# A gated linear attention and two dense layers: attention outputs from block two on in 64x64 array tiles, packed into x by DMAs, and low parts of weight pieces moved to VectorE

## What is computed

```python
for t in range(S):
    state = alpha[:, :, t, :, None] * state + einsum('bhd,bhe->bhde', k[:, :, t], v[:, :, t])
    y[:, :, t] = einsum('bhd,bhde->bhe', q[:, :, t], state)
x = y.transpose(0, 2, 1, 3).reshape(B * S, H * D)
x = mish-like gate of (x @ w_in), times w_out      # h * tanh(softplus(h))
x = (x @ w_in2) * cos(x @ w_in2), times w_out2
```

## Time and profile before

| | |
|---|---|
| median of 3 runs | 884.51 us |
| profiled execution | 883.49 us, span 881.8 us |
| PE busy | 869.1 us, 99% of the span |
| DVE, ACT, POOL busy | 437.2, 405.6, 367.9 us |
| mean granted TensorE clock | 0.998 |
| HBM traffic | 64 GB/s over the span |

### The profile page before, as it was taken

The page is one execution under the profiler, slowest core; times in us unless marked ns, Lnnn a source line. Parts: engine busy times, 40 slices in busy tenths (PEclk is TensorE's granted clock), DMA queues, the critical chain, the costliest instruction groups (busy, mean ns, idle before and its releaser), DMA issues.

```text
span 881.8 us, 16421 instructions
## 1 busy us (share of the span) xinstructions
PE 869.1 (99%) x6614; PEld 719.2 (82%) x6614; DVE 437.2 (50%) x674; ACT 405.6 (46%) x697; POOL 367.9 (42%) x283
## 2 busy tenths in 40 slices
PE   8989999999999999999999999999999999999998
PEld 7768888888888888888888788888888888888886
DVE  8895533333433333320022766665666666666564
ACT  3634333232223223223454765655656556565554
POOL 3786654444455444342455333332333323233232
PEclk9999999999999999999999999999999999999999
DMA  9646543334334333510233200200200200200000
GB/s 222 197 111 161 137 103 72 83 67 110 83 63 108 72 80 66 122 33 1 69 129 90 72 1 1 72 0 1 72 1 1 72 1 1 72 1 1 36 1 36
DMA packets 65611, 57.79 MB, mean 66 GB/s; under 512 B 41952, under 2 KB 51168, under 8 KB 65536
## 3 DMA queue, kind: packets, MB, share of 16 engines
q1 hardware_dynamic: 65536, 56.75, 24.7%
HBM read 42.57 MB, written 14.16 MB: 64 GB/s over the span
## 4 chain that ended last, share of the span: by engine, by line
PE 93%; DVE 4%; issue 1%; ACT 1%; DMA 0%; POOL 0%; ACTq 0%; DVEq 0%; POOLq 0%
PE low L569 43%; PE low L546 33%; PE pair L546 11%; PE top L506 1%; DVE suffix L772 1%; PE top L487 1%; PE pair L439 1%; PE top L492 1%; PE low L466 1%; DVE w_lo L861 1%; DVE growth L783 1%; DMA shared<-aqk_in 0%; DVE probs L816 0%; ACT w_hi L621 0%; PE pair L466 0%
## 5 line engine op out<-in xcount | busy, mean ns | idle before, releaser
L981 POOL TENSOR_TENSOR g_lo<-g,g_hi 128x512 fp32r<-128x512 f32 x192 | 260.4, 1357 | 465.0 <-ACT g_hi L671 465.0
L569 PE MATMUL low<-g_hi,w_hi 128*128 128x512 f32 x576 | 224.6, 390 | 0.3 <-DVE x_out L877 0.3
L569 PE MATMUL low<-g_hi,w_lo 128*128 128x512 f32 x576 | 224.1, 389 | 0.0
L671 ACT ACTIVATE g_hi<-g 128x512 fp32r<-128x512 f32 x192 | 120.7, 628 | 117.6 <-PE low L569 116.8
L569 PE MATMUL low<-g_lo,w_hi 128*128 128x512 f32 x576 | 165.7, 389 | 0.0
L569 PEld LDWEIGHTS low<-g_hi,w_hi 128*128 128x128 f32 x576 | 108.1, 188 | 23.7 <-DVE x_out L877 0.7
L569 PEld LDWEIGHTS low<-g_lo,w_hi 128*128 128x128 f32 x576 | 108.1, 188 | 22.6
L569 PEld LDWEIGHTS low<-g_hi,w_lo 128*128 128x128 f32 x576 | 108.1, 188 | 22.3
L546 PE MATMUL low<-x_hi,w_hi 128*128 128x512 f32 x432 | 124.7, 397 | 0.4 <-ACT x_hi L635 0.3
L546 PE MATMUL low<-x_hi,w_lo 128*128 128x512 f32 x432 | 122.0, 391 | 0.0
L546 PE MATMUL low<-x_lo,w_hi 128*128 128x512 f32 x432 | 121.4, 389 | 0.0
(11 more groups left out here) (108 smaller groups left out, 912.3 us busy)
## 6 DMA issues: line engine op xcount, KB each, us to landing
w_raw<-w_in SPq DMA_DIRECT2D x32, 384.0 KB, 3.3
shared<-aqk_in SPq DMA_DIRECT2D x44, 192.0 KB, 3.8
v_sb<-v_in SPq DMA_DIRECT2D x24, 256.0 KB, 4.3
shared<-aqk_in SPq DMA_DIRECT2D x48, 96.8 KB, 2.7
turned<-x_out SPq DMA_DIRECT2D x72, 64.0 KB, 1.8
kd_t<-turned SPq DMA_DIRECT2D x72, 64.0 KB, 2.4
mid<-x_out SPq DMA_DIRECT2D x6, 768.0 KB, 5.0
shared<-mid SPq DMA_DIRECT2D x6, 768.0 KB, 5.6
```

Of the source, the lines that this page charges most:

```text
L569: mm = nc.tensor.matmul(acc[m], wp[:, f, DM + m * P:DM + (m + 1) * P], gp[:, tile % GB, :], start=(f == 0 and n == 0), stop=(f == FT - 1 a ...
L671: nc.scalar.activation(g_hi[:, tile % GB, :], g[:, tile % GB, :], ACT.Copy).then_inc(ghi_ready, 1)
L981: nc.gpsimd.tensor_tensor(g_lo[:, tile % GB, :], g[:, tile % GB, :], g_hi[:, tile % GB, :].bitcast(F32), ALU.subtract).then_inc(glo_ready, 1)
```

## The change

From chunk 4 on y is no longer made in the row order of x. `inner` (probs times v of each half, 16 matmuls) and `from_states` (states times q, 16 matmuls) each use 64x64 array tiles, one head a tile, into banks 5 and 6; a state is 112 x 48 with the two heads one below the other and no zero blocks; `halves_update` writes the whole 112 rows, so `add_first`, `add_second` and `start_state` are one operation each. The scores go to banks 1 and 7, the updates to banks 0 and 7 (0 is also the bank of h, so `halves_update` waits for g of the step before). y is read out by three operations on ACT (`keep_y_hi`) and three on DVE (`keep_y_lo`), and `pack` moves it into x with 6 DMAs for each part, 12 a chunk, in SP's list around the loads of chunk c + 2. `first_product(16 j)` waits for those DMAs. The array of v and the rows of w_in are in another order to match; for chunks 0 to 3 `values` keeps its 16 matmuls of 32 columns with other tiles. The turned keys' blocks stand in the second half of `probs` and wait for no store of x_out any more.

The visits of block two are at steps 3, 7, 10, 13, then 17, 21, ... 77. A chunk is prepared two steps after the visit of chunk c - 2, one step later than before; the visit of chunk 4 stands ahead of `first_product(3)`, not behind it. `lo_owner` gives pieces 4 to 15 to DVE, and DVE makes keys and queries of chunks 4 and 5.

The core of the diff (left out: semaphores, the removed lines of `values`, other buffers' places, waits that only follow the new counts, the host's arrays):

```diff
+def visit_step(c):
+
+    if c < 2 * BATCH:
+        return (3, 7, 10, 13)[c - BATCH]
+    return FT * (c // BATCH - 1) + 1 + PER_CHUNK * (c % BATCH)
+
+
+VISITED = {visit_step(c): c for c in range(BATCH, CHUNKS)}
...
-    n = s + FT - 3
-    if s >= 3 and n % PER_CHUNK == 0 and n // PER_CHUNK < CHUNKS:
-        return n // PER_CHUNK
-    return None
+    return VISITED.get(s)
...
-    c = values_at(s - 1)
+    c = values_at(s - 2)
...
-    return int(piece in (1, 3, 8, 9, 12, 13) or (piece >= FT and piece % 2 == 1))
+    return int(piece in (1, 3) or 4 <= piece < FT or (piece >= FT and piece % 2 == 1))
...
-        state = sb("state", [P, BATCH, PAIRS, 2 * D])
-        mid_state = sb("mid_state", [P, PAIRS, 2 * D])
+        state = sb("state", [P, BATCH, PAIRS, D])
+        mid_state = sb("mid_state", [P, PAIRS, D])
+        y_hi = sb("y_hi", [P, PAIRS, P], F32R)
+        y_lo = sb("y_lo", [P, PAIRS, P], F32R)
...
+            if c >= BATCH:
+                return banks[1][:, 0:PAIRS * HALF], banks[7][:, 0:PAIRS * HALF]
...
-            return (banks[1][:, 0:PAIRS * D], banks[6][:, P * 2:P * 2 + PAIRS * D])[half]
+            return (banks[0][:, 0:PAIRS * D], banks[7][:, P * 2:P * 2 + PAIRS * D])[half]
+
+        def y_rows(half, i):
+
+            return slice(64 * (i ^ half), 64 * (i ^ half) + D)
...
+            def pack(c, y, x, ready, landed):
+
+                j, b = c // BATCH, c % BATCH
+                sp.wait_ge(ready, c + 1)
+                to, y = x[:, j % 2, :, b * P:(b + 1) * P].bitcast(F32), y[:, :, :].bitcast(F32)
+                for i in range(2):
+                    sp.dma_start(to[D * i:D * i + D, :, :], y[64 * i:64 * i + D, 0:KT, :]).then_inc(landed, 16)
+                sp.dma_start(to[96:128, 0, :], y[0:32, KT, :]).then_inc(landed, 16)
+                sp.dma_start(to[96:112, 1, :], y[32:D, KT, :]).then_inc(landed, 16)
+                sp.dma_start(to[112:128, 1, :], y[64:80, KT, :]).then_inc(landed, 16)
+                sp.dma_start(to[96:128, 2, :], y[80:64 + D, KT, :]).then_inc(landed, 16)
...
+                if c is not None:
+                    pack(c, y_hi, x_hi, xhi_ready, xhi_in)
                 if c is not None and c + 2 < CHUNKS:
                     load_a(c + 2)
                     load_qk(c + 2)
                     load_v(c + 2)
+                if c is not None:
+                    pack(c, y_lo, x_lo, xlo_ready, xlo_in)
...
-                pe.wait_ge(sum_ready, 2 * min(c, UPDATES))
-                if c >= BATCH + 1:
-                    pe.wait_ge(mid_ready, 2 * (c - BATCH))
+                pe.wait_ge(sum_ready, min(c, UPDATES))
+                pe.wait_ge(g_ready, visit_step(c))
...
+                last = 2 * KT
+                parts = [(n, k, h, w) for k in range(KT) for n, h, w in (
+                    (0, 2 * k, 0), (1, 2 * k, 1), (2, 2 * k + 1, 1), (3, last + k // 2, (k + 1) // 2))]
+                parts += [(1, 0, 1, 0), (3, 1, last + 1, 0), (1, 1, 3, 0), (1, 2, 5, 0)]
+                for i, (n, k, h, w) in enumerate(parts):
+                    mm = nc.tensor.matmul(turn[32 * n:32 * n + 32, k * P:(k + 1) * P],
+                                          v_sb[:, c % 3, h, 32 * w:32 * w + 32], probs_of(c, h % 2)[:, h // 2, :],
+                                          start=(i < 4), stop=True, skip_group_check=True)
...
+            def inner(c):
+
+                pe.wait_ge(probs_ready, 2 * (c + 1))
+                pe.wait_ge(v_in_sem[c % 3], 16 * (c // 3 + 1))
+                pe.wait_ge(xhi_ready, c)
+                pe.wait_ge(xlo_ready, c)
+                for p in range(PAIRS):
+                    for half in range(2):
+                        t = slice(HALF * half, HALF * half + HALF)
                         for i in range(2):
...
+                            mm = nc.tensor.matmul(pair[y_rows(half, i), half, p * HALF:(p + 1) * HALF],
+                                                  v_sb[t, c % 3, 2 * p + i, 16 * i:16 * i + D],
+                                                  half_probs[t, i, p, :], start=(p == 0), stop=False,
+                                                  skip_group_check=True)
+                mm.then_inc(inner_done, 1)
...
+            def from_states(c):
+
+                pe.wait_ge(inner_done, c - BATCH + 1)
+                pe.wait_ge(decayed, c - BATCH + 1)
+                pe.wait_ge(mid_ready, c - BATCH + 1)
+                for p in range(PAIRS):
+                    for half, ahead in enumerate((state[:, c % BATCH, :, :], mid_state[:, :, :])):
+                        t = slice(HALF * half, HALF * half + HALF)
+                        for i in range(2):
+                            rows = slice(64 * i, 64 * i + D)
+                            mm = nc.tensor.matmul(pair[y_rows(half, i), half, p * HALF:(p + 1) * HALF],
+                                                  ahead[rows, p, :], q_of(c)[rows, p, t], start=False, stop=True,
+                                                  skip_group_check=True)
+                mm.then_inc(y_done, 1)
 
             def first_product(s):
...
+                if f == 0 and 0 < j < BLOCKS:
+                    pe.wait_ge(xhi_in, 96 * BATCH * j)
+                elif f == 0:
...
-                if c is not None and c > BATCH:
+                if c is not None:
                     halves_update(c)
+                    inner(c)
                     if next_scores(c) is not None:
                         scores(next_scores(c))
-                    values(c)
+                    from_states(c)
                 if alive(s):
                     first_product(s)
                 if scores_at(s) is not None:
                     turn(scores_at(s))
                     scores(scores_at(s))
-                if c == BATCH:
-                    halves_update(c)
-                    values(c)
...
+            def keep_y_hi(c):
+                act.wait_ge(y_done, c + 1)
+                if c > BATCH:
+                    act.wait_ge(xhi_in, 96 * (c - BATCH))
+                    act.wait_ge(xlo_ready, c)
+                for here, rows, half in ((0, slice(0, ROWS), 0), (0, slice(64, ROWS), 1), (64, slice(0, D), 1)):
+                    n = rows.stop - rows.start
+                    mm = nc.scalar.activation(y_hi[here:here + n, :, HALF * half:HALF * half + HALF],
+                                              pair[rows, half, 0:PAIRS * HALF].rearrange("d (p t) -> d p t", p=PAIRS),
+                                              ACT.Copy)
...
+                        nc.vector.tensor_tensor(half_probs[:, i, :, :], score_banks(c)[i].rearrange(
+                            "s (p t) -> s p t", p=PAIRS), causal_half[:, None, :].to_broadcast([P, PAIRS, HALF]),
+                            ALU.mult).then_inc(probs_ready, 1)
...
-                for i in range(2):
-                    rows, cols = slice(64 * i, 64 * i + D), slice(D * i, D * i + D)
-                    nc.vector.tensor_tensor(mid_state[rows, :, cols], update_of(c, 0)[rows, :].rearrange(
-                        "d (p e) -> d p e", p=PAIRS), state[rows, c % BATCH, :, cols], ALU.add).then_inc(mid_ready, 1)
+                nc.vector.tensor_tensor(mid_state[0:ROWS, :, :], update_of(c, 0)[0:ROWS, :].rearrange(
+                    "d (p e) -> d p e", p=PAIRS), state[0:ROWS, c % BATCH, :, :], ALU.add).then_inc(mid_ready, 1)
...
+            def keep_y_lo(c):
+                dve.wait_ge(xhi_ready, c + 1)
+                if c > BATCH:
+                    dve.wait_ge(xlo_in, 96 * (c - BATCH))
+                for here, rows, half in ((0, slice(0, ROWS), 0), (0, slice(64, ROWS), 1), (64, slice(0, D), 1)):
+                    n = rows.stop - rows.start
+                    t = slice(HALF * half, HALF * half + HALF)
+                    mm = nc.vector.tensor_tensor(y_lo[here:here + n, :, t], pair[rows, half, 0:PAIRS * HALF].rearrange(
+                        "d (p t) -> d p t", p=PAIRS), y_hi[here:here + n, :, t].bitcast(F32), ALU.subtract)
+                mm.then_inc(xlo_ready, 1)
...
-                    if c == BATCH:
-                        shrink(c + 1)
-                        grow(c + 1)
-                    keep_x_lo(c)
                     if next_scores(c) is not None:
                         mask(next_scores(c))
                     if c < UPDATES:
                         add_second(c)
+                    keep_y_lo(c)
                 piece = split_at(s)
                 if piece is not None and lo_owner(piece) == 1:
                     split_w(piece)
                 c = prepared_at(s)
-                if c is not None and c > BATCH + 1:
+                if c is not None:
                     shrink(c)
+                    if c == BATCH + 1:
+                        keys(c)
                     grow(c)
+                    if c == BATCH + 1:
+                        queries(c)
...
-                keys(c)
-                queries(c)
-                if c >= BATCH:
-                    decay_state(c)
```

(4 more changed lines are left out.)

173 lines of the change are left out of this document (62 added, 111 removed).

## The result

The change makes the kernel slower. Medians in the same series: 884.14 us before (883.68 to 884.71, 4 runs), 894.94 us after (892.21 to 898.64, 4 runs); ratio 1.0125, 95% interval 1.0086 to 1.0164. Forecast were 876.0 us and a range up to 883. The profiled execution took 895.97 us, its span is 894.2 us.

What follows compares the result with a forecast made beforehand. PE was taken as the bound (busy 99% of the span, 93% of the chain). Terms -15.9 + 0.65 + 1.7 - 4.75 + 4.7 + 5.1 = -8.5 us on 883.49: 875.0 profiled, 876.0 median, range 868 to 883.

Steps and rivals of the forecast that it cites:

- term 6: Chunk 7 (step 13): PE waits 3.6 us for the turned keys behind SP's list, 1.5 for the clock; +5.1 us.
- the pack at a block's end: Moving the last chunk's x_lo at five block ends: hidden with 2.5 us of cover, costed at nothing.
- Rival C: SP's packs become the bound at block ends and chunk 7; slower, about 896 us at 0.9 a pack; chance 0.10.
- Term 1: The visit on PE: scores, inner and from_states at 0.44 us each, 0.81 us less a visit; -15.9 us in sum.
- Rival B: In from_states two row tiles take turns at one bank, 0.88 us instead of 0.44; 884.8 us; chance 0.12.
- Term 2: Before the loop: values of chunks 0 to 3 has six matmuls on column tile 1 instead of four; +0.65 us.
- Term 3: Chunk 4: PE waits 1.85 us for DVE's mask, sum 0.5 later, a 0.63 us gap goes; +1.7 us.
- Term 4: Chunk 5: the 3.46 us wait and slow clock go as POOL makes fewer low parts, 0.3 wait left; -4.75 us.
- Term 5: Chunk 6 (step 10): PE waits 3.4 us for chunk 7's scores, scans behind piece 12's low part, clock 1.3; +4.7 us.

Runs made afterwards that it cites:

- e2: The changed kernel with the five loads of chunk c + 2 ahead of both packs in SP's list, all packs kept; 887.15 us.
- e1: The changed kernel with one DMA a pack instead of six, leaving part of the work out, plus two memsets on POOL at the start; 885.2 us.
- h2: g2 with twelve packs a chunk instead of eight and kd_t's DMAs behind the visit's loads; 3.7 us faster than without that move (886.45 us).
- h4: h2 with the second layer's first four weight pieces loaded at step 32; gains 1.9 us over h2.
- f1: e2 with a chunk prepared one step after the visit of chunk c - 2, as before the change, instead of two; ends at e2's time.
- f3: f1 with high and low parts of y and of x in one buffer each, so 8 pack DMAs a chunk instead of 12; 5 us faster.
- g4: The changed kernel with only the low parts of pieces 4, 5, 9, 12 and 15 made later; 893.75 us.
- h3: g2 with kd_t's DMAs behind the visit's loads and the second layer's first four weight pieces loaded at step 32; 876.20 us, ratio 0.9904.
- g1: f3 with the low parts of pieces 9, 12 and 15 made one step later, behind the visit's y_lo; 881.44 us.
- g2: g1 with the low parts of pieces 4 and 5 also made later, behind chunk 4's y_lo; time equal to g1.
- f2: f1 with chunk 4's visit at step 4 instead of 3, behind first_product(3); 3.8 us slower than f1.

## Why the prediction was wrong

- **The step that failed.** It is SP's list: term 6, and the pack at a block's end that was costed at nothing. I priced SP's new DMAs by rows of other transfers (0.45 us a pack, 1.8 us for the blocks to land) and carried nothing of SP's lag into the next block. Measured were 0.65 us a pack, up to 4.6 us for the landing, 5.5 us more than forecast at chunk 7 and 4.0 us at the beginning of block three. e2 shows the list as the cause: another order of the same DMAs gives 7.8 us back. 21.0 us lie between the forecast (8.5 faster) and the profiled execution (12.5 slower); the rest of it is 2.5 at chunk 4, 2.5 at chunk 6, 1.9 at chunk 8, 2.3 for the visits of chunks 9 to 23, and pieces under 1.5 us.
- **Rival C** (SP's packs become the bound, 0.10) was the nearest, in part. It had chunk 7 right in kind. Of its five waits at a block's beginning one came. At the measured pack its rule gives chunk 7 2.4 us more and the blocks nothing (12 x 0.20 - 2.5 is below 0), so still 6.1 us faster than before: it priced only the packs' own length, not that SP's list carries its lag on. That its example of 896 us lies beside the measured 894.94 is luck; it took a pack at 0.9.
- **Term 1** (visit): right in kind, too large. `inner`, scores and `from_states` follow each other at 0.48 and 0.50 us, not 0.44; a visit saves 0.66 to 0.71, not 0.81 (period 18.56 for 19.22). That is 0.15 x 15 = 2.3 us of the miss in chunks 9 to 23. Rival B (two row tiles taking turns at a bank) is refuted: its records start between 226.00 and 226.45 us, the 0.45 us that the 16 scores take with a bank for each row tile. The Trainium skill, page "TensorEngine Tiling (Array Packing)", section "Restrictions and Gotchas", says that different row tiles cannot access the same PSUM bank at once; here the trace disagrees, 0.45 us where turns would have taken 0.88, for row tiles that also stand in different column tiles.
- **Term 2** (before the loop): right, +0.67 us at the first product and +0.5 from s=1 on.
- **Term 3** (chunk 4): the wait for the mask has the size of the forecast (1.75 for 1.85), though both of its ends came about 1.2 us later than I had them. Missed was the wait for the scores, 1.47 us: I let it vanish with the turn at POOL, but DVE's own growth and queries took 2.79 and 1.50 us beside POOL's work. Behind the two waits the clock was down, which I had left open at 0.9. +3.4 for +0.9.
- **Term 4** (chunk 5): right, -5.1 for -5.6. The wait was 1.04 us, not 0.3, and the clock stayed up; that the term still came out within 0.5 is partly luck.
- **Term 5** (chunk 6): a wait of the forecast size at the forecast place (4.09 for 3.4), for another reason. SP's loads of chunk 7 were issued last at 74.06, behind kd_t's DMAs and six packs. The reason I gave was there behind it: e1 and e2 free SP and still show 4.24 us, with DVE's growth (2.16 us there, beside POOL's keys, for 1.23 here) and POOL's queries directly ahead. The slow clock cost some 2.9 us, not 1.3.
- **Term 6** (chunk 7): the right releaser, the wrong size: 7.79 us for 3.6. Its own rows add up to 17.4, so to a wait of 4.0, not 3.6. The list of SP was right row by row; but twelve packs took 7.8 us for 5.4, and the last block landed after 4.6 us instead of 1.8. The 1.8 is a median over the whole trace before. With a load of weights directly ahead the blocks took 2.3 to 2.8 us there too (60.1 to 61.5 us), and here one load of weights, five of inputs and six packs had been issued in the 7.1 us before. h2 and h4 show what loads of weights ahead of the blocks cost in landing, 3.7 for 1.8 us. The slow clock behind the wait cost some 2.7 us, not 1.5.
- **Costed at nothing: the pack at a block's end.** The cover of 2.5 us did not hold at block three's beginning. SP came to the packs at 190.12, behind the blocks (183.02) and kd_t's DMAs (188.05), 3.3 us after ACT had made y_hi (185.65 + 1.17); and twelve packs took 2.4 us more. The wait was 2.16 us and about 1.8 more at the lower clock. The later blocks held. In the f kernels f1 to f3 and in the g and h kernels except g4 the wait for x came at the beginning of block two instead (0.7 to 6.2 us).

What stays open: chunk 8's kd_t wait of 1.74 us was seen only as SP's lag running on, and no run treats it alone. The 0.88 us at 339.08 (chunk 19) stand in the middle of `from_states`, where the program waits for nothing; like the 1.8 us in h3 they have no releaser in the profile, and nothing shows that SP has to do with them. Why the last of the four blocks in the changed kernel took 4.6 us when the other three took 2.6 to 2.9 is not settled either.

## What to carry to other kernels

Cost a queue as a resource with its own in-order list, down to what stands in front of each wait: an issue that waits for a landing holds every load behind it, and two edits of order here (loads ahead of packs; kd_t's DMAs behind the loads) gave 7.8 and 4.6 us without one instruction less. Take the price of a new DMA from no other DMA's row when its shape is new, and a landing from a row with the same transfers ahead of it; carry both ends through every place where the queue returns. When a removed wait doesn't pay (g1, g2), look for what paces the loop, rather than for the next wait.

## What the runs showed that I had not expected

- An SBUF to SBUF copy of 16 to 48 partitions occupies its issuing queue for 0.59 to 0.64 us, on SP and on ACT (0.62) alike; the DMAs of the blocks and of kd_t, between SBUF and DRAM, take 0.44 and 0.51 (medians of L332 and L338).
- On ACT these issues stop the engine's own work: 3.40 us for six.
- The DMAs of the blocks land 1.6 us to 4.6 (the changed kernel) or 6.0 us (h3) after their issue. With three loads of weights directly ahead it was 3.7 us, without them 1.8 (medians in h2 and h4).
- A low part on DVE takes 0.93 to 4.14 us by what POOL does beside it.
- After a wait of 2.16 us the granted clock was 0.50 in the changed kernel and 1.00 in f2; after 1.4 to 1.5 and 1.1 us in close succession it was 0.50 in h2 (40 to 42 us) and 1.00 in g2. The length of the wait alone does not tell. In the changed kernel, at 40 to 42 and at 204 to 206 us PE was busy throughout at the lower level.
